# The logits of the second routing: x tiles kept in free places of the weight buffer, one group of twelve tiles, sums written instead of added

## Chip, core and metric

The kernel runs on one core of one Trainium2 chip (trn2). The metric is the device time of one execution in microseconds (us), lower is better. The engines are TensorE (PE, with its weight loads as PEld), VectorE (DVE), ScalarE (ACT), GpSimd (POOL) and SyncE (SP); SP issues most DMAs, POOL all indirect ones.

## What is computed

Attention, then two mixtures of experts, on N = 1536 tokens of D = 512 values, E = 8 experts, FF = 1024 hidden units, all in float32. Only the passage between the two mixtures matters here:

```
x1 = first mixture (each token goes to its two best experts):
     x1[n] = sum over its two experts e of gate[n, e] * (relu(x[n] @ w1[e]) @ w2[e])
second mixture, on x1:
     compute = x1 @ w_skip > 0
     logits  = x1 @ w_gate            (8 per token; with the skip score 9)
     e       = argmax(logits);  gate = softmax(logits)[e]
     out     = x1 + gate * (relu(x1 @ w1'[e]) @ w2'[e])   where compute, else x1
```

So the second routing needs nine numbers of every token of the finished x1, and the second mixture can't gather its first tokens before the lists of that routing are made.

## The kernel before

**Tiling.** P = 128 partitions, NT = 12 tiles of 128 tokens. In the second routing tile t holds the tokens 12p + t (partition p), so a tile is a strided read of x1. Weights of one expert are 16 chunks of 128 x 512 values (WC = 16), cut in PIECES = 8 pieces of 512 KB. SP loads a piece into its place in the buffer `stage` (L571, `load_piece`, at most AIR = 4 in flight), ACT rounds it into `w_hi` (L1097) and DVE subtracts to get `w_lo` (L1615, which counts `s_lo`); only then may that place of `stage` be loaded again. Two sets `w_hi`/`w_lo` alternate. Sets 0 to 7 belong to the first mixture, set 8 is the first of the second mixture and set 9 its second. When the first mixture ends, set 8 is rounded and split, and set 9 lies unrounded in `stage`; it is rounded during the first slots of the second mixture (L1097, L1615 there).

**First mixture.** Experts in order, in rounds of up to W = 416 tokens (parts of 128, 128, 128 and 32); here every expert has one round. A round computes the hidden units (L850), then the output transposed, 128 columns at a time (L856). Each of these four chunks is copied by ACT into `out_t` (L1221), turned back by PE (`turn_y`, L839) and scaled by DVE into `rows_out` (L1855, L1861). In the last expert's rounds `turn_y` also multiplies `out_t` by the second router's weights (L831), which gives the part of the second logits that this last expert adds; DVE scales it into `more_out` (L1844). POOL's `put` sends per round, first, four indirect DMAs of 36-byte rows from `more_out` to the DRAM array `x_more` (L1429, with add), then four of full rows from `rows_out` to `x1_dram` (L1441, with add), and waits for all to land. In rounds of other experts `more_out` is zero.

**The x tiles of the second routing.** Once all experts but the last are put into x1 (wait on `yfree`), SP copies x1 in DRAM to `x_part` (L616, 4 DMAs), lets the last expert's rows be added to `x1_dram` (`s_may_put`), and loads the tiles one by one from `x_part` into `rows_in` (L635), the gather buffer of the first mixture, four places round. That can only start when the last round's gathers are used up, and from tile 4 on each load waits until PE has turned the tile that was there. Before the load of tile 11, SP waits for the sums in `x_more` and loads them as `more_logit` (L631). The last half (4 pieces) of set 9 is loaded after the copy to `x_part`.

**Logits.** For each tile PE turns 128 x 512 values (L1059, 4 transposes into a bank), ACT copies them to `xt_b` (L1174), PE multiplies with the nine router columns as the stationary operand and 128 tokens as the moving one (L768), which gives 9 x 128, ACT copies that to `gt_sb` (L1182) and PE turns it to 128 x 9 (L775). DVE adds `more_logit` (L1683) and runs some 21 small operations (`route`, L1683 to L1766, and `totals`, L1643 to L1653). The order is: PE `ranks` (L786, L791) once `mask_b` (L1723) is there, DVE ranks to lanes and columns, then per tile a lane mask `lane_hot` (DVE L1776, or ACT L1163 and L1156 for the tiles in `by_act`) and `col_val` (DVE L1778), and PE `lists` (L804) sums their product over the tiles. This is done in two groups of six tiles: the first group's DVE work lies beside the logits of the second. ACT stores the gates of each group into x1_dram (L1143), after `s_m1done`, which POOL gives when the first mixture's last rows have landed.

**Start of the second mixture.** DVE casts the lists (L1785), POOL gathers the first slot's rows (L1537, into `xg`), while PE runs ten warm-up matmuls (`keep_warm`, L693); then PE turns the slot (L936), and the matmuls of the slot follow (L964). SP issues four copies of x1 to the output (L642), and POOL the gather of the second slot (L1508). `keep_busy(n, ...)` (L687) is n transposes with no use but to keep PE active.

## Time and profile before

| | us |
|---|---|
| median of 3 runs | 666.77 (666.35 to 667.37) |
| the profiled execution, its own time | 665.87 |
| its span | 663.4 |
| PE busy | 620.8 (94% of the span) |
| DVE busy | 367.9 (55%) |
| ACT busy | 293.9 (44%) |
| POOL busy | 237.9 (36%) |

The span is what the trace covers; the rest of 665.87 lies around it. "Busy" of PE counts matmuls that overlap. In the rows below a time is in us from the start of the span, a mean or a minimum of one instruction in ns. "x4" is a number of instructions, "<-" names who ended an idle time before an instruction.

### The profile page before, as it was taken

To read this page: it belongs to the slowest core of one execution; us is meant where nothing else is said; L and a number is where in the kernel's file an instruction comes from. 1 tells how busy PE (TensorE), PEld (TensorE's weight loads), DVE (VectorE), ACT (ScalarE), POOL (GpSimd) and SP (SyncE) were. 2 spreads that over 40 slices of the span, in tenths; PEclk is the share of its full clock that TensorE was granted. 3 is DMA by queue.
4 is the path that set the end of the run, shared out by engine and by line. 5 is a ranking of instruction groups with operands and counts; after the bars stand their busy time and mean duration, and the time that the engine had idled before them with its cause. 6 is when DMAs were issued, how large, how long until landed. Compare 5 with 4: busy or idle time off the path is not lost.

```text
span 663.4 us, 13555 instructions
## 1 busy us (share of the span) xinstructions
PE 620.8 (94%) x4054; PEld 551.5 (83%) x4054; DVE 367.9 (55%) x714; ACT 293.9 (44%) x536; POOL 237.9 (36%) x223
## 2 busy tenths in 40 slices
PE   6888848999999999999999999998699999999994
PEld 6567735999999999999999999985478888888883
DVE  5759985644535554364644536423564687656641
ACT  2657732433424443253433434433255475646621
POOL 2558303105527063370725527033112223231230
PEclk9999967999999999999999999998699999999998
DMA  9999881442926448283672926885296679568220
GB/s 305 326 285 305 301 295 53 155 152 55 269 66 180 140 93 264 54 213 94 150 207 54 273 65 157 236 251 113 72 330 208 208 220 357 160 187 266 40 50 13
DMA packets 57633, 119.79 MB, mean 181 GB/s; under 512 B 13588, under 2 KB 13972, under 8 KB 57568
## 3 DMA queue, kind: packets, MB, share of 16 engines
q1 hardware_dynamic: 39424, 94.59, 43.4%
q0 software_dynamic: 14304, 23.93, 17.2%
q10 hardware_dynamic: 3840, 0.49, 0.5%
q8 instruction: 30, 0.49, 0.3%
q14 instruction: 35, 0.29, 0.1%
HBM read 103.51 MB, written 23.50 MB: 191 GB/s over the span
## 4 chain that ended last, share of the span: by engine, by line
PE 84%; DMA 5%; DVE 4%; issue 2%; SPq 2%; POOLq 0%; ACT 0%; POOL 0%; DVEq 0%; ACTq 0%
PE bank L964 22%; PE bank L856 22%; PE bank L850 22%; PE bank L839 2%; DMA q_ring<-in_q 2%; PE bank L819 2%; PE bank L745 2%; PE bank L980 2%; PE bank L724 1%; DMA xg<-x_moe,ix_take 1%; PE bank L768 1%; PE bank L758 1%; PE bank L713 1%; PE bank L936 1%; DVE col_val L1778 1%
## 5 line engine op out<-in xcount | busy, mean ns | idle before, releaser
L1615 DVE TENSOR_TENSOR w_lo<-stage,w_hi x120 | 141.7, 1222 | 22.9 <-ACT w_hi L1097 22.1
L1097 ACT CAST w_hi<-stage x120 | 119.7, 1050 | 9.0 <-PE bank L964 8.9
L856 PE MATMUL bank<-unit_hi,w_hi 128*128 128x416 f32 x256 | 92.6, 362 | 0.0
L1873 DVE SCALAR_TENSOR_TENSOR unit_lo<-bank,unit_hi 128x416 fp32r<-128x416 f32 x64 | 37.9, 592 | 96.8 <-ACT unit_hi L1211 96.8
L850 PE MATMUL bank<-tok_hi,w_hi 128*128 128x416 f32 x256 | 90.5, 354 | 0.6 <-DVE tok_lo L1825 0.6
L1211 ACT ACTIVATE unit_hi<-bank 128x416 fp32r<-128x416 f32 x64 | 33.2, 519 | 129.9 <-PE bank L850 129.9
L856 PE MATMUL bank<-unit_lo,w_hi 128*128 128x416 f32 x256 | 90.2, 352 | 0.0
L850 PE MATMUL bank<-tok_hi,w_lo 128*128 128x416 f32 x256 | 89.7, 350 | 0.0
L856 PE MATMUL bank<-unit_hi,w_lo 128*128 128x416 f32 x256 | 89.7, 350 | 0.0
L1429 POOL DMA_INDIRECT x_more<-more_out,ix_put x32 | 51.6, 1614 | 42.2 <-DVE more_out L1844 26.3
L1441 POOL DMA_INDIRECT x_moe<-rows_out,ix_put x32 | 55.2, 1726 | 9.8 <-issue 9.8
L850 PE MATMUL bank<-tok_lo,w_hi 128*128 128x416 f32 x256 | 58.5, 350 | 0.0
L1409 POOL COPY ix_take<-take_ix 128x4 int32 (+1 forms) x8 | 1.5, 184 | 135.2 <-PE bank L819 135.2
L850 PEld LDWEIGHTS bank<-tok_hi,w_hi 128*128 128x128 f32 x256 | 48.0, 188 | 1.5 <-issue 1.0
L856 PEld LDWEIGHTS bank<-unit_hi,w_hi 128*128 128x128 f32 x256 | 48.1, 188 | 1.0
L856 PEld LDWEIGHTS bank<-unit_hi,w_lo 128*128 128x128 f32 x256 | 48.3, 189 | 0.5
L850 PEld LDWEIGHTS bank<-tok_hi,w_lo 128*128 128x128 f32 x256 | 48.1, 188 | 0.4
L856 PEld LDWEIGHTS bank<-unit_lo,w_hi 128*128 128x128 f32 x256 | 48.0, 188 | 0.4
L850 PEld LDWEIGHTS bank<-tok_lo,w_hi 128*128 128x128 f32 x256 | 47.9, 187 | 0.5
L964 PE MATMUL bank<-w_hi,ht_hi 128*128 128x512 f32 x112 | 46.7, 417 | 0.0
L964 PE MATMUL bank<-w_hi,xt_hi 128*128 128x512 f32 x112 | 45.6, 407 | 0.5 <-ACT xt_hi L1254 0.5
L964 PE MATMUL bank<-w_lo,ht_hi 128*128 128x512 f32 x112 | 44.3, 395 | 0.0
(162 smaller groups left out, 1072.5 us busy)
## 6 DMA issues: line engine op xcount, KB each, us to landing
stage<-in_moe_w SPq DMA_DIRECT2D x128, 512.0 KB, 5.6
v_win<-in_v SPq DMA_DIRECT2D x24, 198.0 KB, 8.9
v_raw<-in_v SPq DMA_DIRECT2D x6, 528.0 KB, 13.4
x_moe<-rows_out SPq DMA_DIRECT2D x12, 260.0 KB, 3.6
kt<-in_k SPq DMA_DIRECT2D x8, 384.0 KB, 9.0
q_ring<-in_q SPq DMA_DIRECT2D x6, 512.0 KB, 9.6
x_att<-x_sb POOLq DMA_DIRECT2D x12, 256.0 KB, 5.8
x_part<-x_moe SPq DMA_DIRECT2D x4, 768.0 KB, 8.8
```

The lines of the kernel that those rows point to most:

```text
L745: last = eng.matmul(ps_heads[part, h, 0:HD + 1], pt_sb[:, s % 2, i, part], v_win[:, (2 * t + half) % WR, h * VD:(h + 1) * VD], start=True, ...
L819: last = eng.transpose(ps[:, i * rows:(i + 1) * rows], rows_in[0:rows, t, i * P:(i + 1) * P], ident[0:rows, 0:rows])
L839: last = eng.transpose(ps_turn[0:PART[t], t * P:(t + 1) * P], out_t[:, PSTART[t]:PSTART[t] + PART[t]], ident)
L850: last = eng.matmul(ps_unit[f % 2][:, 0:W], w, x, start=(i == 0), stop=(i == len(mine) - 1))
L856: last = eng.matmul(ps_out[chunk][:, 0:W], w[:, WC // 2 + f, chunk * P:(chunk + 1) * P], h[:, f % UNITS, :], start=(f == 0 and i == 0), st ...
L964: last = eng.matmul(ps[:], *every[i], start=(i == 0), stop=(i == len(every) - 1))
L1097: eng.copy(piece(w_hi[n % SETS], j), stage[:, j, :]).then_inc(s_hi, 1)
L1211: eng.activation(unit_hi[:, f % UNITS, :], ps_unit[f % 2][:, 0:W], ACT.Relu)\
L1429: eng.indirect_dma_start(more_dram, bass.IndirectOffsetOnAxis(ap=ix_put[0:rows, t:t + 1], axis=0), more_out[0:rows, t, :], None, bounds_ch ...
L1441: eng.indirect_dma_start(x1_dram, bass.IndirectOffsetOnAxis(ap=ix_put[0:rows, t:t + 1], axis=0), rows_out[0:rows, t, :], None, bounds_chec ...
L1615: eng.tensor_tensor(piece(w_lo[n % SETS], j), stage[:, j, :], piece(w_hi[n % SETS], j).bitcast(F32), ALU.subtract)\
L1873: eng.scalar_tensor_tensor(unit_lo[:, f % UNITS, :], ps_unit[f % 2][:, 0:W], 0.0, unit_hi[:, f % UNITS, :].bitcast(F32), ALU.max, ALU.subt ...
```

## The change

1. `x_part` is gone, with its four copies. `x1_sb` now lies in places 0 to 5 of `stage` (two tiles in each), which are free from the moment when set 8 is split. SP loads the twelve tiles with six DMAs directly from `x1_dram`, while the last expert's round is computed; `s_may_put` is given when they have landed. Then SP waits for the sums and loads `more_logit`. All eight pieces of set 9 are loaded after that, each of the first six when PE has turned the two tiles in its place.
2. PE turns tiles 0 and 1 in the place of the 8 `keep_busy` transposes ahead of the last `turn_y`; the other 8, behind it, are gone.
3. The logits are computed with the 128 tokens as the stationary operand and the nine router columns as the moving one, straight into 128 x 9. The copy to `gt_sb` and the second turn are gone.
4. One group of twelve tiles instead of two of six; ACT makes `lane_hot` for the six odd tiles, DVE for the even ones. 16 `keep_busy` transposes stand between the last logits and `ranks`.
5. The indirect DMAs to `x_more` write plainly, without add.

```diff
-        ps_rank, ps_list, ps_x1 = bank[1], bank[0], (bank[6], bank[0])
+        ps_rank, ps_list, ps_x1 = bank[1], bank[0], bank[0:2]
...
-        x1_sb = rows_in[:, :, 0:D]
+
+        X1_PIECES = NT * D // (PC * D)
+        x1_sb = stage[:, 0:X1_PIECES, :].rearrange("p j (t d) -> p (j t) d", d=D)
...
-        GROUPS = (((0, NT),), ((0, NT // 2), (NT // 2, NT)))
+        GROUPS = (((0, NT),), ((0, NT),))
...
-        by_act = [2 * t + 1 for t in range(NT)] + [2 * NT + t for t in range(GROUPS[1][1][0], NT, 2)]
+        by_act = [2 * t + 1 for t in range(NT)] + [2 * NT + t for t in range(1, NT, 2)]
...
-            for g in range(PIECES, ready):
-                if g == ready - PIECES // 2:
-                    land(0)
-
...
-                    eng.wait_ge(round_sems["yfree"],
-                                eng.snap(total, min_val=0, max_val=E * ROUNDS) + 1)
-                    for rows in base_rows:
-                        eng.dma_start(part_dram[rows, :], x1_dram[rows, 0:D]).then_inc(s_part, 16)
+            last_set = ready - PIECES
+            for g in range(PIECES, last_set):
                 load_piece(g)
                 land(AIR - 1)
-            eng.wait_ge(s_part, 16 * BASES)
+            land(0)
+
+            eng.wait_ge(s_counted, 1)
+            eng.reg_load(counts, todo_i[0:1, 0:E])
+            eng.reg_mov(total, 0)
+            for e in range(E - 1):
+                eng.reg_add(total, total, counts[e])
+
+            eng.wait_ge(round_sems["yfree"], eng.snap(total, min_val=0, max_val=E * ROUNDS) + 1)
+            by_tile = x1_dram.rearrange("(p t) d -> p t d", t=NT)
+            per = NT // X1_PIECES
+            for i in range(X1_PIECES):
+                eng.wait_ge(s_lo, last_set + i - 2 * PIECES + 1)
+                eng.dma_start(x1_sb[:, i * per:(i + 1) * per, :], by_tile[:, i * per:(i + 1) * per, 0:D])\
+                   .then_inc(s_x1[i], 16)
+            for i in range(X1_PIECES):
+                eng.wait_ge(s_x1[i], 16)
             eng.sem_inc(s_may_put, ROUNDS)
             eng.reg_add(total, total, counts[E - 1])
-            eng.wait_ge(round_sems["xtp"],
-                        eng.snap(total, min_val=0, max_val=E * ROUNDS) * PARTS + (PARTS + 1))
-
-            for t in range(NT):
-                if t == NT - 1:
-
-                    all_rounds = eng.snap(total, min_val=1, max_val=E * ROUNDS)
-                    for part in range(PARTS):
-                        eng.wait_ge(s_put_sums[part], all_rounds * 16)
-                    eng.dma_start(more_logit[:], more_dram.rearrange("(p t) e -> p t e", t=NT))\
-                       .then_inc(s_more, 16)
-                if t >= XR:
-                    eng.wait_ge(s_x1t, t - XR + 1)
-                eng.dma_start(x1_sb[:, t % XR, :], part_dram.rearrange("(p t) d -> p t d", t=NT)[:, t, :])\
-                   .then_inc(s_x1[t % XR], 16)
+            all_rounds = eng.snap(total, min_val=1, max_val=E * ROUNDS)
+            for part in range(PARTS):
+                eng.wait_ge(s_put_sums[part], all_rounds * 16)
+            eng.dma_start(more_logit[:], more_dram.rearrange("(p t) e -> p t e", t=NT)).then_inc(s_more, 16)
+            for g in range(last_set, ready):
+                if g - last_set < X1_PIECES:
+                    eng.wait_ge(s_x1t, (g - last_set + 1) * per)
+                load_piece(g)
+                land(AIR - 1)
...
+            def turn_tile(t):
+                if t % per_piece == 0:
+                    eng.wait_ge(s_x1[t // per_piece], 16)
+                if t >= 2:
+                    eng.wait_ge(s_x1te, t - 1)
+                for i in range(DK):
+                    last = eng.transpose(ps_x1[t % 2][:, i * P:(i + 1) * P],
+                                         x1_sb[:, t, i * P:(i + 1) * P], ident)
+                last.then_inc(s_x1t, 1)

...
             def second_logits(t):

-                if t >= 2:
-                    eng.wait_ge(s_gte, t - 1)
                 for i in range(DK):
-                    last = eng.matmul(gt_place(t)[0:E + 1], wgate2[:, i, :], xt_b[t % 2][:, i, :],
-                                      start=(i == 0), stop=(i == DK - 1))
-                last.then_inc(s_gt[1], 1)
-
-            def turn_logits(t):
-
-                eng.wait_ge(s_gte, t + 1)
-                eng.transpose(second_place(t, t + 1), gt_sb[:, t % 2, :],
-                              ident[0:E + 1, 0:E + 1]).then_inc(s_gl, 1)
+                    last = eng.matmul(second_place(t, t + 1), xt_b[t % 2][:, i, :], wgate2[:, i, :],
+                                      start=(i == 0), stop=(i == DK - 1), skip_group_check=True)
+                last.then_inc(s_gl, 1)
...
-                keep_busy(8, ps_unit[0])
+                for t in range(2):
+                    turn_tile(t)
...
-            keep_busy(8, ps_unit[0])
             eng.wait_ge(s_xt_idle, 1)
-            first, second = GROUPS[1]
-            for t in range(NT + 2):
-                if t < NT:
-                    eng.wait_ge(s_x1[t % XR], 16 * (t // XR + 1))
-                    if t == 2:
-                        eng.wait_ge(s_xt_idle, 2)
-                    if t >= 2:
-                        eng.wait_ge(s_x1te, t - 1)
-                    for i in range(DK):
-                        last = eng.transpose(ps_x1[t % 2][:, i * P:(i + 1) * P],
-                                             x1_sb[:, t % XR, i * P:(i + 1) * P],
-                                             ident)
-                    last.then_inc(s_x1t, 1)
-                if t == first[1] + 4:
-                    ranks(1, first)
-                if 1 <= t <= NT:
+            for t in range(NT):
+                if t >= 2:
+                    turn_tile(t)
+                if t:
                     eng.wait_ge(s_x1te, t)
                     second_logits(t - 1)
-                if t >= 2:
-                    turn_logits(t - 2)
-            lists(1, first)
-            ranks(1, second)
-            lists(1, second)
+            eng.wait_ge(s_x1te, NT)
+            second_logits(NT - 1)
+            eng.wait_ge(s_xt_idle, 2)
+            keep_busy(16, ps_turn)
+            for group in GROUPS[1]:
+                ranks(1, group)
+                lists(1, group)
             second_mixture()
...
-            first, second = GROUPS[1]
             weights(0, GROUPS[0][0])
             store_gates(0, GROUPS[0][0])
             lanes(0, GROUPS[0][0])
             first_mixture()
-            for t in range(NT + 1):
-                if t < NT:
-                    empty_x1(t)
-                if t:
-                    empty_gt(t - 1)
-                if t == first[1] + 3:
-                    weights(1, first)
-
+
+            eng.wait_ge(s_xt_idle, 1)
+            for t in range(NT):
+                empty_x1(t)
+            weights(1, GROUPS[1][0])
             eng.wait_ge(s_m1done, 1)
-            store_gates(1, first)
-            weights(1, second)
-            store_gates(1, second)
-            lanes(1, second)
+            store_gates(1, GROUPS[1][0])
+            lanes(1, GROUPS[1][0])
             second_mixture()
...
-                                               oob_is_err=False, compute_op=ALU.add)\
-                           .then_inc(s_put_sums[t], 16)
+                                               oob_is_err=False).then_inc(s_put_sums[t], 16)
```

## Rows read from the trace of the kernel before

**Rows 1.** The chain of waits in order of time: start, length, what
```profile
438.72 0.59 PE bank L839 x4
...
442.33 0.59 PE bank L1059 x4
442.92 0.97 PE bank L768 x8
...
450.39 5.81 DMA more_logit<-x_more
...
472.66 4.55 PE bank L693 x10
...
479.88 9.24 DMA xg<-x_moe,ix_take
```

**Rows 2.** Timeline of DVE: start, length, line, operation [idle before <-releaser]
```profile
456.31 0.21 DVE L1683 TENSOR_TENSOR logit<-bank,more_logit 128x54 f32<-128x54 f32 x1 [16.11 <-DMA more_logit<-x_more]
...
458.15 0.21 DVE L1723 TENSOR_TENSOR mask_b<-hot,chosen 128x48 bf16<-128x48 f32 x1
...
464.66 0.21 DVE L1683 TENSOR_TENSOR logit<-bank,more_logit 128x54 f32<-128x54 f32 x1 [1.69 <-PE bank L775]
...
468.65 0.17 DVE L1764 SCALAR_TENSOR_TENSOR lane_f<-block_f,rank_f 128x6 f32<-128x6 f32 x1
...
469.65 0.32 DVE L1778 TENSOR_SCALAR col_val<-column_h,col_f,c_late 128x128 f16<-128x128 f16 x1
...
471.26 0.31 DVE L1778 TENSOR_SCALAR col_val<-column_h,col_f,c_late 128x128 f16<-128x128 f16 x1
```

**Rows 3.** Windows: length; PE, PEld, DVE, ACT, POOL busy; then PEclk, DMA share, GB/s
```profile
471.90:477.60 5.70, 4.94 (x15) 3.68 (x14) 1.16 (x4) 0.00 (x0) 1.10 (x1) 0.55 0.17 47
```

**Rows 4.** Timeline of SP: the copies to x_part, all four
```profile
419.42 2.66 SPq L616 DMA_DIRECT2D x_part<-x_moe  x4
```

**Rows 5.** The page's DMA issues: KB each, median us from issue to landing
```profile
stage<-in_moe_w SPq DMA_DIRECT2D x128, 512.0 KB, 5.6
```

**Rows 6.** Timeline of PE in the attention: the first router's logits, and what follows
```profile
47.61 0.96 PE L758 MATMUL bank<-wgate,xt_a 128*128 128x16 f32 x8
48.51 0.69 PE L745 MATMUL bank<-v_win,pt_sb 120*64 120x65 f32 x16
```

**Rows 7.** Timeline of POOL between the mixtures
```profile
440.40 1.56 POOL L1429 DMA_INDIRECT x_more<-more_out,ix_put  x1 [24.02 <-DVE more_out L1844]
...
446.00 1.33 POOL L1429 DMA_INDIRECT x_more<-more_out,ix_put  x1 [0.30 <-issue]
...
453.24 1.33 POOL L1441 DMA_INDIRECT x_moe<-rows_out,ix_put  x1 [0.30 <-issue]
473.28 1.10 POOL L1537 DMA_INDIRECT xg<-x_moe,take_ix  x1 [18.71 <-DVEq L1786]
```

**Rows 8.** POOL's gathers of one line: duration ns min/median/max, first and last start
```profile
L1415 POOL DMA_INDIRECT rows_in<-x_att,ix_take x32: 933/1020/1118, 115.1 to 397.6; - x32
```

**Rows 9.** DVE's reduction of one line at two widths, the same columns
```profile
L1734 DVE TENSOR_REDUCE den<-top_e x2: 202/202/202, 458.5 to 466.8; 128x6 f32<-128x48 f32 x2
L1734 DVE TENSOR_REDUCE den<-gates x1: 252/252/252, 91.8 to 91.8; 128x12 f32<-128x96 f32 x1
```

**Rows 10.** Timeline of DVE, first routing: the first and last of twelve such entries
```profile
96.52 0.53 DVE L1778 TENSOR_SCALAR col_val<-column_h,col_f,c_late 128x128 f16<-128x128 f16 x2
...
103.21 0.52 DVE L1778 TENSOR_SCALAR col_val<-column_h,col_f,c_late 128x128 f16<-128x128 f16 x2
```

**Rows 11.** Timeline of ACT, first routing: its first lanes and the fifth relu
```profile
95.29 0.69 ACT L1163 ACTIVATE lane_hot<-lane_h,lane_f 128x128 f16<-128x128 f16 x2 [4.47 <-DVE lane_f L1764]
...
98.34 0.29 ACT L1156 ACTIVATE lane_hot<-lane_hot 128x128 f16<-128x128 f16 x1
```

**Rows 12.** DMA issues from 445 to 490 us, without a size
```profile
x_moe<-rows_out,ix_put POOLq DMA_INDIRECT x4, 6.7
...
xg<-x_moe,take_ix POOLq DMA_INDIRECT x1, 3.5
```

More of the change, by code:

```diff
@@ L306, in build @@
         col_f = sb_in(routing, "col_f", [P, 2, NT])
-        gt_sb = sb_in(routing, "gt_sb", [E + 1, 2, P])
-        XR = PARTS
         second = ExitStack()
@@ L359, in build @@
         s_xst = [sem(f"s_xst{i}") for i in range(2)]
-        s_gt = [sem(f"s_gt{m}") for m in range(2)]
+        s_gt = sem("s_gt")
         s_z = sem("s_z")
@@ L385, in build @@
         s_lo = sem("s_lo")
-        s_x1 = [sem(f"s_x1{i}") for i in range(XR)]
+        s_x1 = [sem(f"s_x1{i}") for i in range(X1_PIECES)]
         BASES = 4
```

27 lines of the change are left out of this document (6 added, 21 removed).

## Prediction, made before the changed kernel was run

> **What bounds the kernel now.** The page has PE busy for 94% of the span, so inside the two mixtures nothing off PE is worth anything. The change touches only the passage between them, and there I read the chain of waits in order of time [rows 1]. The last turn of the first mixture ends at 438.72 + 0.59 = 439.31 us. Then come eight idle transposes, tiles (0.59 to turn one, 0.97 for its logits), the wait for the sums of the last expert (`more_logit`, issued at 450.39, 5.81 on the way), and more tiles. The timeline of DVE gives the joints [rows 2]: the first group starts at 456.31, when `more_logit` has landed, the second at 464.66, behind the last tile; its last `col_val` ends at 471.26 + 0.31 = 471.57. From there to the second mixture runs a fixed tail: ten warm-ups that end at 477.21 [rows 1], beside the first gather. The passage so far takes 471.57 - 439.31 = 32.3 us, and the question is when the last `col_val` ends. In the tail PE is granted 0.55 of full speed, so mostly the lower level, 1.2 GHz [rows 3], after a stretch in which it waited for DVE; it will wait so again, and I leave the tail as it is.
>
> **Loading the tiles.** The copies to `x_part` start at 419.42 [rows 4], as soon as the rows of the round before the last are in x1. The six new loads wait for the same, and for six pieces of set 8 to be split, which the last round does early. They are as large as weight pieces, 512 KB, of which four in flight take 5.6 us each [rows 5]: six need 8.4 us and are down at 428; at twice that at 436.3. PE asks for tile 0 ahead of the last `turn_y`, at 437. I take no wait; the range allows 1 us. The twelve single loads, and SP's waits for PE among them, go. Moved in exchange: all eight pieces of set 9, four of which were loaded long before, are now issued behind `more_logit`, from about 449. By the same row they need 11.2 us and are down at 460; at twice that at 471.5. Set 9 is first needed in the slots, after that; behind the pieces SP only holds the copies to the output, which wait for the first gather anyway. POOL's queue gets nothing new.
>
> **The turns.** Tiles 0 and 1 take the place of the first eight idle transposes, eight for eight: nothing. The second eight go; what they cost lies ahead of the tiles. ACT empties both tiles beside `turn_y`.
>
> **The tiles.** The second turn and its copy go, a turn stays 0.59. The logits now load 128 columns of tokens and move nine. The nearest row is the first router, tokens stationary with 16 moving columns: its eight instructions hold PE from 47.61 to 48.51, 0.90 us [rows 6]. The old form, 0.97, is the upper bound; below I allow 0.25, as if only the moving columns shrank (0.97 x 9/128 = 0.07) and the rest were starts. With 0.90, 12 x 0.90 + 10 x 0.59 = 16.7 us: the last logits end at 439.31 + 16.7 = 456.0 and DVE can start at 456.05. With 0.97 it is 456.9. The Trainium skill ("TensorE: Matmul & The Clock Gate", Back-to-back issue gap) gives matmuls of up to 64 moving columns some 60 cycles; by that alone a tile's eight cost about 0.2 us, an estimate from that page of the Trainium skill, and the tiles would end near 448. The 0.90 of the first router speaks against it.
>
> **The sums.** The first put to `x_more` starts at 440.40, the fourth at 446.00, 1.87 apart [rows 7]. No plain indirect write is in the trace. Above it is bounded by that put with add; below by POOL's gathers, 1.02 us [rows 8], plus the 0.30 between two. I take the gather, which like the new write has no add: the fourth starts at 440.40 + 3 x 1.32 = 444.4. Landing and SP's step took at most 450.39 - 446.00 = 4.4, and `more_logit` 5.8 (it now shares the DMA engines with pieces instead of tiles): the sums are there at 454.6; with the old pitch at 456.2. So this part by itself is worth at most 0.1; what goes is SP's order, which held `more_logit` behind eleven tile loads.
>
> **One group.** DVE starts once, at 456.05, and not at 464.66: 8.6 earlier. But the work that lay beside the tiles is now bare. The second group took 471.57 - 464.66 = 6.91. Twelve tiles widen some 11 operations from 48 to 96 values per partition, 50 ns each by the two widths of one reduction [rows 9], and two from 90 to 180, some 94 each: 0.74 in all. The masks of six tiles took 471.57 - 469.65 = 1.92; twelve go at the pace of the first routing, where two `col_val` and a `lane_hot` take (103.21 - 96.52) / 11 = 0.61 [rows 10], so 6 x 0.61 = 3.66, or 1.74 more. Sum 6.91 + 0.74 + 1.74 = 9.39, and the last `col_val` ends at 465.4. The 16 idle transposes last at most 4 x 0.59 = 2.4 us, to 458.4; `mask_b` came 2.05 after the start of its group (456.31 to 458.36 [rows 2]) and comes with 0.35 of the widening at 458.45: hidden, barely. A faster tile chain doesn't shift that, as both start together.
>
> **ACT's lanes.** ACT waits for `s_m1done` ahead of the gates and, queued behind them, all six lanes, which PE's lists need (three before, when the rows had long landed). `lane_f` is there at 456.05 + (468.82 - 464.66) + 0.74 = 461.0. In the first routing the fifth relu came 3.05 after the first lane [rows 11]; with a sixth it is some 3.6, so ACT is done at 464.6, with 0.8 to spare. `s_m1done` comes with the last row put, issued at 453.24 [rows 7]; such puts take 6.7 [rows 12]. With quicker sum puts it is issued 1.6 earlier, at 451.6, and lands at 458.3: in time, unless pieces slow it by over 2.7 + 0.8.
>
> **The sum.** 471.57 - 465.44 = 6.1 us less, the tail unchanged. Against the profiled execution: 665.87 - 6.1 = 659.8. The median of the runs is 0.9 above that execution, so the forecast is 666.77 - 6.1 = 660.7. With logits at 0.97, or 1 us lost on a tile, it is 661.6 to 661.7, with both 662.6; with the sums deciding at 454.6, 659.3.
>
> **Rivals.**
> *The pieces get in the way, in part.* They fly from 449 on beside the row puts, the store of the gates and perhaps the first gather (new start 473.28 - 6.1 = 467.2 [rows 7]). For it: the second slot's gather, beside the output copies, took 9.24 [rows 1] where the first took 3.5 [rows 12]. The Trainium skill's rule ("DMA: Bandwidth & Descriptors", Queues, rings and completion order), that each DMA engine goes round the queues that have work, speaks against the change here; those two rows agree with it. Price: a put that lands 5.5 us late costs 2; a gather of 5.5 costs 2. So 662.7 to 664.7. Chance 0.16.
> *The moving columns set the pace* (the case of the Trainium skill's rule): a tile costs 0.59 + 0.25, the tiles end at 448.2, and DVE waits for the sums, 454.6. Gain 6.1 + 1.4 = 7.5: 659.3. For it: so few columns; against it: rows 6. Chance 0.06.
> *Slower: the pieces take over the tail.* At twice their time they fly until 471.5. The last put takes twice its 6.7 and lands at 465.0, the six lanes end at 468.6, 3.2 late, and the first gather takes 9.24, 5.7 more. Together 8.9 against 6.1: 669.6. It decides where such delays pass 6.1. Against it: by their usual time the pieces are down at 460. Chance 0.05.
> *No change.* The bare DVE chain is longer than its sum, or the first tile is late, by the whole 6.1, so that the cover given up equals the start won: 666.8. The first routing, with twice the picks, shows nothing of the kind. Chance 0.03.
>
> **How the numbers follow.** The forecast's own case has 0.70, from 659.3 to 662.6. The range takes in the fast rival with 0.5 for its error and most of the first slow one: 658.8 to 664.2, which leaves out the end of that one, no change, the slower case, and a rest of the own case: 0.2. What a measurement of this kernel can tell from no change is about 0.2%, 1.3 us. Faster by more than that: 0.70 + 0.06 + 0.13 = 0.89; within 0.03 + 0.03 = 0.06; slower 0.05.
>
> **What would show it.** Right: logits at 0.90 a tile, PE without idle to 456; `more_logit` landed before that; one L1683 at 456, its idle ended by PE; puts to `x_more` near 1.0 us each; the last `col_val` at 465.4; the first gather at 467, in 3.5 us. Wrong: L1683 released by a DMA, a first lane on ACT after 461.8, PE waiting for ACT in the lists, or a gather above 5 us.

## The result, and the profile after

The changed kernel took 670.34 us in the median of 11 executions (666.92 to 674.64), the kernel before 665.08 beside it (11 executions, 662.16 to 668.41): ratio 1.0075, 95% interval 1.0052 to 1.0097. That is slower by some 5 us where 6.1 faster was forecast, and outside the range. Ratios here leave out executions more than 1.5% above the fastest of their kernel; that is none of these eleven, but one to three executions in each of five kernels below (`add`, `busy1_add`, `busy2_again`, `busy2_end8`, `early_nine2`), while the medians count all. The profiled execution took 666.92 us, the fastest of the eleven; from its page, and below it the same line of the kernel before:

```profile
span 664.8 us, 13461 instructions
...
PEclk9999967999999999999999999995699999999998
```
```profile
PEclk9999967999999999999999999998699999999998
```

A slice is 664.8 / 40 = 16.6 us; the passage between the mixtures lies in slices 27 to 29 (432 to 482). In slices 28 and 29 the granted clock falls to 5 and 6 tenths, where the kernel before has 8 and 6. The changed kernel in stretches (columns: length; PE, PEld, DVE, ACT, POOL busy; PEclk, DMA share, GB/s):

```profile
440.00:446.00 6.00, 5.59 (x53) 5.36 (x51) 0.00 (x0) 2.34 (x4) 4.63 (x5) 1.00 0.02 2
...
448.00:450.00 2.00, 0.54 (x3) 0.54 (x3) 0.00 (x0) 1.07 (x2) 1.70 (x2) 0.67 0.76 197
450.00:456.00 6.00, 6.00 (x31) 6.00 (x31) 0.00 (x0) 1.17 (x2) 1.95 (x2) 0.50 1.07 334
456.00:462.00 6.00, 6.00 (x31) 6.00 (x31) 0.00 (x0) 1.17 (x2) 0.00 (x0) 0.50 0.70 208
462.00:466.00 4.00, 4.00 (x22) 3.99 (x22) 2.76 (x14) 0.28 (x1) 0.00 (x0) 0.53 0.85 326
```

Up to 446 the clock is 1.00, from 450 to 462 exactly 0.50, the lower of its two levels (1.2 GHz), although PE is busy all of 450 to 462. The chain of waits (start, length, what), against [rows 1]:

```profile
439.01 0.80 PE bank L767 x8
439.80 0.49 PE bank L760 x4
...
445.42 0.41 issue
...
446.88 1.92 PE bank L760 x4
448.82 0.59 ACT xt_b L1157
...
452.28 1.51 PE bank L767 x8
453.79 0.94 PE bank L760 x4
...
462.86 3.27 PE bank L677 x16
...
473.75 4.60 PE bank L683 x10
```

A tile cost 0.80 + 0.49 = 1.29 us at first. Then two waits came (445.42 and, inside the 1.92 of 446.88, the one that ACT's copy at 448.82 ends), and from there 1.51 + 0.95 = 2.46 a tile. ACT's timeline shows the waits from the other side, with what ended its idle time in brackets:

```profile
440.33 0.58 ACT L1157 COPY xt_b<-bank 128x512 f32<-128x512 f32 x1 [1.79 <-PE bank L760]
...
442.98 0.58 ACT L1157 COPY xt_b<-bank 128x512 f32<-128x512 f32 x1 [0.79 <-PE bank L760]
445.19 0.58 ACT L1157 COPY xt_b<-bank 128x512 f32<-128x512 f32 x1 [1.62 <-PE bank L760]
448.82 1.07 ACT L1157 COPY xt_b<-bank 128x512 f32<-128x512 f32 x2 [3.05 <-PE bank L760]
```

ACT waited 3.05 us for a turn that PE had begun at 444.79 and that takes 0.6: the completion reached ACT some 3 us late. The copy before it, at 445.19, was already some 1 us late. DVE, SP and POOL, against [rows 2, 4, 7]:

```profile
462.89 0.27 DVE L1652 TENSOR_TENSOR logit<-bank,more_logit 128x108 f32<-128x108 f32 x1 [22.99 <-PE bank L767]
...
465.10 0.26 DVE L1692 TENSOR_TENSOR mask_b<-hot,chosen 128x96 bf16<-128x96 f32 x1
...
467.88 0.17 DVE L1733 SCALAR_TENSOR_TENSOR lane_f<-block_f,rank_f 128x12 f32<-128x12 f32 x1
...
472.09 0.53 DVE L1747 TENSOR_SCALAR col_val<-column_h,col_f,c_late 128x128 f16<-128x128 f16 x2
```
```profile
417.56 3.18 SPq L612 DMA_DIRECT2D stage<-x_moe  x6
446.10 0.33 SPq L621 DMA_DIRECT2D more_logit<-x_more  x1
446.56 14.52 SPq L562 DMA_DIRECT2D stage<-in_moe_w  x8
```
```profile
440.16 1.03 POOL L1399 DMA_INDIRECT x_more<-more_out,ix_put  x1 [25.36 <-DVE more_out L1813]
...
444.10 0.88 POOL L1399 DMA_INDIRECT x_more<-more_out,ix_put  x1 [0.30 <-issue]
445.28 1.59 POOL L1410 DMA_INDIRECT x_moe<-rows_out,ix_put  x1 [0.30 <-issue]
...
474.32 1.09 POOL L1506 DMA_INDIRECT xg<-x_moe,take_ix  x1 [22.07 <-DVEq L1755]
```

The last `col_val` ends at 472.09 + 0.53 = 472.62, where the forecast had 465.4 and the kernel before 471.57.

The fastest execution understates the loss. Each execution lists its mean granted clock: in the changed kernel's eleven it runs from 0.961 (666.92 us) down to 0.947 (672.11 us) and 0.948 (674.64 us), median 0.951; the kernel before had medians of 0.970 to 0.972 in the later comparisons (21 to 35 executions each). So, on the whole, the executions that lost more time are those that lost more clock.

### The profile page after: what moved, and what is told of

It is laid out like the page before. It is cut to its first block, busy times and chain, and to the rows that moved or that the text cites. A ratio compares the mean times of both kernels' runs of the same rounds, so it can differ in the third digit from the quotient of the medians.

```text
span 664.8 us, 13461 instructions
## 1 busy us (share of the span) xinstructions
PE 622.7 (94%) x4036; PEld 559.4 (84%) x4036; DVE 366.4 (55%) x690; ACT 291.9 (44%) x529; POOL 220.2 (33%) x223
## 4 chain that ended last, share of the span: by engine, by line
PE 87%; DVE 4%; DMA 4%; issue 2%; SPq 1%; ACT 0%; POOLq 0%; POOL 0%; DVEq 0%; ACTq 0%
PE bank L958 22%; PE bank L849 22%; PE bank L843 22%; PE bank L832 2%; PE bank L767 2%; PE bank L812 2%; PE bank L736 2%; PE bank L974 2%; PE bank L715 2%; DMA v_raw<-in_v 2%; PE bank L704 2%; DMA xg<-x_moe,ix_take 1%; PE bank L760 1%; PE bank L749 1%; DVE col_val L1747 1%
## 5 line engine op out<-in xcount | busy, mean ns | idle before, releaser
L1410 POOL DMA_INDIRECT x_moe<-rows_out,ix_put x32 | 59.3, 1852 | 9.8 <-issue 9.8
L1399 POOL DMA_INDIRECT x_more<-more_out,ix_put x32 | 33.3, 1042 | 43.8 <-DVE more_out L1813 27.8
```

The lines of the kernel that those rows point to most:

```text
L1399: eng.indirect_dma_start(more_dram, bass.IndirectOffsetOnAxis(ap=ix_put[0:rows, t:t + 1], axis=0), more_out[0:rows, t, :], None, bounds_ch ...
L1410: eng.indirect_dma_start(x1_dram, bass.IndirectOffsetOnAxis(ap=ix_put[0:rows, t:t + 1], axis=0), rows_out[0:rows, t, :], None, bounds_chec ...
```

## The experiments

The kernels came in five sets, each on one chip beside the kernel before, so ratios can be compared between sets better than medians. None but `plain_pad` is 2% off the kernel before; the differences below are small ones. "Way" is, within the profiled execution, the time from the start of the last expert's logits to the turn of the first slot's rows; it leaves out what the rest of the program does (before: 437.76 to 477.05, with the clock at 0.5 in 460.0 to 463.4, so rather a long one of its kind). "Clock falls" is its first fall behind 430 us. Clock is the median over all executions of their means.

```
kernel        logits  idle  sums   tile us      late   clock  clock  way    median  ratio, 95% interval
              move    /tile        full (half)  comp.  falls  mean   us     us
before        128     0     add    1.71         no     460.0  0.971  39.29  -       1
changed       9       0     plain  1.29 (2.46)  yes    448.7  0.951  40.72  670.34  1.0075 (1.0052-1.0097)
again         9       0     plain  1.28 (2.45)  yes    446.3  0.956  41.06  668.80  1.0054 (1.0031-1.0076)
late          9       0     plain  1.28 (2.45)  yes    447.3  0.957  40.43  668.41  1.0035 (1.0013-1.0057)
moving128     128     0     plain  1.71         yes    468.5  0.972  37.68  665.51  0.9997 (0.9976-1.0018)
busy4         9       4     plain  1.72 (3.31)  yes    453.8  0.953  48.12  675.91  1.0143 (1.0110-1.0177)
nine_only     9       0     add    1.28 (2.45)  no     455.0  0.957  36.65  666.37  1.0009 (0.9983-1.0035)
add           9       0     add    1.28 (2.45)  no     445.7  0.956  38.07  668.63  1.0015 (0.9982-1.0047)
plain_only    128     0     plain  1.71         yes    468.8  0.970  39.09  667.94  1.0027 (1.0000-1.0054)
stage_only    128     0     add    1.71         no     466.0  0.970  35.91  664.23  0.9988 (0.9961-1.0015)
mov_add       128     0     add    1.71         no     471.0  0.971  36.27  664.76  0.9979 (0.9951-1.0007)
stage_early   128     0     add    1.71         no     461.7  0.970  35.89  664.35  0.9993 (0.9957-1.0029)
busy4_add     9       4     add    1.72         no     464.6  0.970  35.98  664.51  0.9983 (0.9955-1.0012)
busy2_add     9       2     add    1.50         no     459.4  0.972  35.06  661.05  0.9931 (0.9904-0.9959)
busy2_again   9       2     add    1.50         no     465.4  0.969  34.76  663.73  0.9946 (0.9913-0.9979)
busy2_end8    9       2     add    1.50         no     460.6  0.968  34.62  663.75  0.9975 (0.9945-1.0005)
busy1_add     9       1     add    1.39         no     465.1  0.956  34.62  669.50  1.0030 (0.9989-1.0070)
early_nine2   9       2     add    1.50         no     460.9  0.961  35.62  665.89  0.9994 (0.9965-1.0023)
plain_pace    128     0     plain  1.71         no     461.9  0.972  40.39  666.93  1.0013 (0.9985-1.0041)
```

(One more, plain_pad, is told below.) `nine_only`, `plain_only` and the two `plain_pa..` are the kernel before with that part alone; `stage_only`, `stage_early` and `early_nine2` keep its two groups.

**First set.** `again` is the changed kernel once more: 

> The changed kernel once more, for a second profile beside its twins of this call. Theory A (the clock): logits with only nine moving columns load PE so lightly that after its first pause the granted clock falls to 1.2 GHz and doesn't come back in the tiles: a tile costs 2.45 us there, 1.29 at 2.4 GHz. It expects the fall again, at about the same place or earlier, and about 670 us, 5 over the kernel before. Theory B (traffic): PE's pause at 447 to 449 us comes from the weight pieces or the plain puts; it expects a pause at the same distance behind the issue of the pieces. Theory C (one group): the bare DVE chain of 9.6 us is the loss, with the clock only a part of it.

`moving128` puts the old logits back:

```diff
-                    last = eng.matmul(second_place(t, t + 1), xt_b[t % 2][:, i, :], wgate2[:, i, :],
+                    last = eng.matmul(gt_place(t)[0:E + 1], wgate2[:, i, :], xt_b[t % 2][:, i, :],
...
+                eng.transpose(second_place(t, t + 1), gt_sb[:, t % 2, :],
```


> The changed kernel with the logits in the old form (nine columns stationary, 128 tokens moving, copy to gt_sb, second turn); tile loads, one group and plain sums stay. Theory A: the clock stays at 2.4 GHz through the tiles, each costs about 1.6 us, the last logits are ready at 439 + 12 x 1.12 + 10 x 0.5 = 457.5 instead of 462.9, and the kernel is 4 to 6 us faster than the changed one, near the kernel before. Theory B: the pause comes all the same and the time stays near 670. Theory C: the same as the changed kernel.

`busy4` adds idle transposes to the changed kernel's tiles:

```diff
                     second_logits(t - 1)
+                    keep_busy(4, bank[3])
```


> The changed kernel with four idle transposes (128 moving columns each, 0.45 us) behind the logits of each of the tiles 0 to 10. Theory A: the clock holds, a tile costs 1.29 + 0.45 = 1.74, the last logits come at 439 + 17.9 + 0.5 = 459 to 460 instead of 462.9, so 3 us or more faster than the changed kernel though PE does more. Theory B and C: the added work of 5 us comes on top, slower than the changed kernel by 3 to 5 us.

`late` holds the pieces of set 9 back until all rows are in x1:

```diff
+            eng.wait_ge(s_m1done, 1)
             for g in range(last_set, ready):
```


> The changed kernel with the eight pieces of set 9 issued only when the first mixture's last rows are in x1 (about 459 us), so none flies beside the tiles before. Theory B: no pause at 447, the clock holds, DVE starts at 456: 6 us faster. Theory A: the same time as the changed kernel within 1 us, with the same fall of the clock.

`late` kept the late completions and the fall of the clock, so the pieces cause neither; what is left to them is at most the step from 1.0054 to 1.0035, within the intervals. They do stretch the last round's row puts: from issue to landing (median of four) 9.4 us in `again` and 5.1 in `late`, against 6.7 before. That held up nothing here, but it comes back in the fourth set. `moving128` kept the clock at 1.00 through all tiles and gave back the whole loss: from 1.0054 to 0.9997, and 3.3 us of the median where 4 to 6 were expected. Yet `busy4`, which has as much for PE to do, was the slowest of all. Its timeline of PE (start, length, line, operation, idle before):

```profile
451.65 0.60 PE L760 MATMUL bank<-c_late,stage 128*128 128x128 f32 x4
453.93 1.88 PE L767 MATMUL bank<-wgate,xt_b 128*128 128x9 f32 x8 [1.68 <-ACT xt_b L1158]
455.65 1.09 PE L677 MATMUL bank<-c_late 128*128 128x128 f32 x4
```

A late completion held PE for 1.68 us there, and the clock fell at the end of that hold, to 0.5 from 453.8 to 477.7, after which the added work cost double. So it could not tell whether work holds the clock; the late completions had to be taken away first.

**Second set, one part at a time.** `nine_only` is the kernel before with the new form of the logits alone (item 3 of the change), `plain_only` with the plain writes alone:

```diff
-                                               oob_is_err=False, compute_op=ALU.add)\
-                           .then_inc(s_put_sums[t], 16)
+                                               oob_is_err=False).then_inc(s_put_sums[t], 16)
```


> The kernel before with one part of the change alone: the logits with tokens stationary and nine columns moving; the copy to gt_sb and the second turn go; two groups, tile loads from x_part, sums with add stay. Theory A (the light logits lose the clock): the granted clock falls in the tile loop here too, a tile costs 2.45 us after it, and the kernel is 2 to 6 us slower than the one before. Theory D (the late completions of PE, seen in all four kernels with tiles in stage and plain sums, lose the clock): without them the clock holds, a tile costs 1.3 to 1.4 us, PE waits for the sums, and the kernel is 0 to 3 us faster than before.

> The kernel before with plain sums alone. POOL's four puts take 1.0 us each in place of 1.56, but more_logit stays behind the tile loads on SP. Theories A and C: no change of the time (within 0.2%). Theory D with the plain writes as cause: PE's completions come up to 3 us late some 8 us after POOL's first put, a tile is held, and the kernel is 1 to 3 us slower than before.

`add` is the changed kernel with that line the other way round, `stage_only` the kernel before with the tiles in the places of weight pieces:

> The changed kernel with the sums added, as before, in place of plain writes. Theory A: the clock falls at 446 to 449 us all the same, time as the changed kernel within 1.5 us. Theory D with the plain writes as its cause: no late completion (ACT's copies of x_b follow PE's turns by less than 1 us), the clock holds, and the kernel is 5 us or more faster than the changed one.

> The kernel before with the tile loads of the change alone (tiles in stage straight from x1, set 9 behind them, more_logit as soon as the sums are there); old logits, two groups, sums with add. more_logit should be there 2 to 4 us earlier than in the kernel before, so the first group's DVE work lies beside the tiles and no tile waits; the clock holds. Theory A: 2 to 4 us faster than before. Theory D with the tiles in stage as the cause of late completions: a hold of 1 to 3 us at tile 5 or 6, and no gain.

Two causes came apart here. In `add` no completion is late and PE has no pause, and the clock falls all the same (windows as above):

```profile
440.00:446.00 6.00, 6.00 (x56) 6.00 (x56) 0.00 (x0) 2.59 (x5) 5.08 (x4) 0.98 0.20 2
446.00:452.00 6.00, 6.00 (x32) 6.00 (x30) 0.00 (x0) 1.76 (x3) 5.06 (x4) 0.50 0.60 114
452.00:459.00 7.00, 7.00 (x36) 7.00 (x36) 0.00 (x0) 1.17 (x2) 1.33 (x1) 0.50 1.06 327
```

PE is busy 100% at 0.50. The Trainium skill ("TensorE: Matmul & The Clock Gate", HAM oscillation) names gaps in which PE idles as what costs the clock; here the trace shows it lost without a gap, with tiles of nine moving columns. Three of `add`'s twelve executions, 671.9 to 674.2 us, are not in its ratio of 1.0015; the mean of all twelve is 668.18 us, beside 665.97 of the kernel before.

And `plain_only`, with the old logits, has the clock but the late completions. DVE's first logits come 19.85 us behind the start of the last expert's logits instead of 18.55 (458.83 - 438.98, 456.31 - 437.76), the second group's no later than before, and the way is no longer. Its ratio of 1.0027 has an interval that reaches 1.0000, so a cost of the plain writes alone is likely, not shown. An estimate: the profile before spent 1.5 us more on three pieces of its last tiles at half clock (1.81 + 0.92 + 1.29 in its chain, against 0.97 + 0.59 + 0.97 at full), which this one did not, so the late completions may have cost about that; in the one-group kernels with the old logits the way is 37.68 with plain and 36.27 with added sums (`moving128`, `mov_add`).

`nine_only` kept full clock from its first logits (442.49) through nine tiles' logits; it fell at 455.0, in a wait of 2.66 us for the ranks, and the last three logits ran at half. `add` lost it 7.5 us behind its first (438.18 to 445.7). So nine columns without filler do not lose the clock at a fixed point. `nine_only` has all sixteen idle transposes ahead of its tiles, two groups and the old loads; which of these held the clock longer was not tested. Over all its executions the mean clock is 0.957, no better than `add`'s 0.956. `stage_only` was expected 2 to 4 us faster: its way is 3.4 shorter, its median 1.3 lower, and its interval holds 1.

**Third set, both undone, or the clock held by work.** `mov_add` is `moving128` with added sums, `busy4_add` is `busy4` with added sums, and `stage_early` is `stage_only` with tiles 0 and 1 turned ahead of `turn_y`:

```diff
-                keep_busy(8, ps_unit[0])
+                for t in range(2):
+                    turn_tile(t)
```


> The changed kernel with the two suspects undone together: logits again with nine stationary and 128 moving columns and a second turn, and the sums again added instead of written; the tile loads from stage, the early turns of tiles 0 and 1 and the one group stay. Theory A (nine moving columns lose the granted clock) and theory D (the plain writes make TensorE's completions late, about 2 us) together: granted clock 1.00 through all tiles, a tile every 1.7 us without a hold, last turn of logits near 460 in a profile of 666, and the median 0.3 to 0.6% below the kernel before, about 662.5. If a pause at tiles 5 and 6 comes in spite of the added sums, D is wrong, and the time is that of the run with the old logits alone, ratio 1.000. Theory G (the one group is the loss, its chain of 9.4 us on VectorE being bare): the clock as above, but a ratio of 1.000 or more, and a kernel with two groups and the same loads is faster by 1 us or more.

> The kernel before with its tiles loaded from stage and, in addition, tiles 0 and 1 turned ahead of the last turn of the expert's result; old logits, two groups, sums added. The run with the loads alone stood at 0.9988. Two tiles of 1.7 us are in work before the loop instead of eight idle transposes: the first group's logits at VectorE about 2 us earlier than in that run where the logits of the expert part are also there (more_logit issued near 450 stays, so the first group's start can't be below 452), the last group's start about 2 to 3 us earlier. Expected ratio 0.994 to 0.998 by theories A and D. Under theory G this one beats the one-group kernel of the same call; under its rival (one group costs nothing, for the first group's ranks and lists lie between the tiles and hold them up) it is the slower of the two or equal.

> The changed kernel with four idle transposes behind the logits of each tile from 0 to 14, as in the earlier run with them, but with the sums added instead of written: the pause at tiles 5 and 6, ahead of which the clock fell in that run, should be gone. If the clock follows how long TensorE works on matrix columns (theory A1), the four transposes of 128 columns take the place of the old logits' 128 moving columns: clock 1.00 through the tiles at about 1.7 us each, last logits near 459, ratio 0.995 to 1.000. If it falls all the same with no pause in the tiles (theory A2: few moving columns behind full weight loads lower it whatever lies between), it stands at 0.5 from about 446 to 454 on, a tile then takes about 3.3 us as in that run, and the ratio is 1.005 to 1.015.

`busy4_add` is the clean form of `busy4`, and the first of the two cases came: clock 1.00 to the last tile.

```profile
446.00:452.00 6.00, 6.00 (x58) 6.00 (x58) 0.00 (x0) 2.04 (x4) 5.08 (x4) 1.00 0.33 29
452.00:459.00 7.00, 7.00 (x68) 7.00 (x66) 0.00 (x0) 2.35 (x4) 3.14 (x3) 1.00 1.03 299
```

All three stand at a way of 35.9 to 36.3 us and 0.998 to 0.999, each with 1 in its interval; `mov_add` and `stage_early` fell short of what was expected of them. Theory G (the one group costs something) seems to get nothing: 35.89 with two groups, 36.27 and 35.98 with one. But these ways can't decide it. ACT and DVE of `stage_early`:

```profile
463.96 0.24 ACT L1141 ACTIVATE top_e<-top_d 128x48 f32<-128x48 f32 x1 [4.15 <-POOLq L1570]
...
464.31 0.20 DVE L1739 TENSOR_REDUCE den<-top_e 128x6 f32<-128x48 f32 x1 [2.05 <-ACT top_e L1141]
```

ACT stores the first group's gates only when the last row put has landed (`s_m1done`, L1570), and `top_e` of the second group stands behind that store. DVE waits 2.05 us for it, and in the kernel before not at all. So the two-group kernel lost 2.0 us there to another wait; without it, an estimate, its way would be some 2 us shorter than that of the one-group kernels. Theory G stays open.

**Fourth and fifth set, less filler, and the late completions.** `busy2_add`, `busy1_add` have two and one transposes in place of four; `busy2_end8` has eight ahead of the ranks instead of sixteen; `busy2_again` repeats `busy2_add`; `early_nine2` puts nine columns and two transposes into `stage_early`.

> As the run before it with four idle transposes behind each tile's logits and added sums (granted clock 1.00 in all tiles, tile 1.72 us, 35.98 us from the last expert's logits to the turn of the first slot's rows), with two transposes instead of four. Theory A1 leaves open how much work holds the clock: with none it fell at 445.7, with four it held. If two hold it, a tile takes about 1.50 us, the last logits end 2.2 us earlier and the stretch is about 33.8 us, ratio 0.993 to 0.997. If two don't, the clock reads 0.5 from somewhere after 446 on, a tile takes 2.9 us from there, and the stretch is 37 to 40 us, ratio 1.000 to 1.006.

> The kernel before with tiles loaded from stage, tiles 0 and 1 turned early, added sums, two groups, nine-moving-column logits and two idle transposes behind the logits of each tile; the first group's ranks stand behind the last turn of a tile. Its sister with the old logits took 35.89 us from the last expert's logits to the turn of the first slot's rows, the one-group form with the same tile pace 35.98. If the clock holds (theory A1, two suffice) a tile takes 1.50 us and the stretch is about 33.5 us, ratio 0.992 to 0.996, provided that the first group's logits at VectorE (not before 451.5, when the sums' logits are read) leave its lists done before the second group's. If the clock falls it is 37 us or more and the ratio 1.000 or above. Theory G (one group costs something of its own) says that it is faster than busy2_add by over 0.5 us in that stretch; its rival says the two agree within 0.5.

> The one-group kernel with nine-column logits, added sums and one idle transpose a tile; with two it had the clock at 1.00 up to 459.4, a tile in 1.50 us and a stretch of 35.06 us, with none the clock fell at 445.7 (38.07 us). Theory A1 (the clock follows how much TensorE has to do): one lies between. If it holds, a tile takes 1.39 us and the stretch is about 34.0, ratio 0.992; if it falls in the midst of the tiles, 36 to 38 us and a ratio of 0.998 to 1.004.

> The faster version with eight idle transposes ahead of the ranks instead of sixteen. In its profile the sixteen took 3.61 us at the lowered clock and ended at about 462.8, 0.76 us after mask_b (462.03). With eight they end by 461.5, and the ranks follow mask_b at once: stretch 34.3 us instead of 35.06, ratio 0.001 below that of its sister in this call. If instead the clock goes down earlier or stays down longer for the missing work, the slot turn is not earlier, and the ratio is that of the sister or above.

> The one-group kernel with nine-column logits, added sums and two idle transposes a tile once more. Its first runs gave 0.9931 with an interval from 0.9904 to 0.9959, and its profile a stretch 4.2 us shorter than that of the kernel before (35.06 against 39.29), of which the start of the second mixture keeps all: 0.9936. So 0.992 to 0.996 again; a value within 0.2% of 1 would say that the first was luck of the runs.

With two the tile is 1.50 and PE has no wait (timeline of PE in `busy2_add`):

```profile
453.00 0.96 PE L767 MATMUL bank<-wgate,xt_b 128*128 128x9 f32 x8
453.82 0.41 PE L677 MATMUL bank<-c_late 128*128 128x128 f32 x2
454.07 0.60 PE L760 MATMUL bank<-c_late,stage 128*128 128x128 f32 x4
...
458.57 0.96 PE L767 MATMUL bank<-wgate,xt_b 128*128 128x9 f32 x8
459.38 3.61 PE L677 MATMUL bank<-c_late 128*128 128x128 f32 x16
462.79 0.24 PE L779 MATMUL bank<-mask_b,before_b 128*128 128x96 bf16 x1
...
476.14 0.81 PE L930 MATMUL bank<-c_late,xg 128*128 128x128 f32 x4 [0.56 <-DMA xg<-x_moe,take_ix]
```

Both sets of executions put it below both kernels, 0.9931 and 0.9946. But it is not safe: three of the twelve executions of `busy2_again`, which its ratio leaves out, took 675 to 676 us at a mean clock of 0.945 to 0.948. The mean of all twelve is 666.07 us, beside 665.71 of the kernel before, so nothing is gained there; in `busy2_add` no execution is left out, and the means are 661.41 and 665.75. With one transpose the profiled execution kept the clock and had a way of 34.62, yet the median of all was 669.50 at 0.956: most lost it.

The ways fell less than the tiles. In `busy2_add` the last `col_val` ends 5.4 us earlier in the way than before (28.40 against 33.81), but the way is only 4.2 shorter, 35.06 where 33.8 was expected. The chain that ended last there no longer runs over PE and DVE:

```profile
456.60 8.75 DMA x_moe<-rows_out,ix_put
...
465.99 5.62 DMA x_moe<-gates
...
472.62 3.48 DMA xg<-x_moe,take_ix
...
476.14 0.82 PE bank L930 x4
```

The last row put lands, only then ACT stores the gates, and the first gather waits for that store. The puts take 9.4 us beside the pieces of set 9 (median of four), so here the pieces do get in the way. `busy2_again`, `busy2_end8` and `busy1_add` have the same chain. That is why `busy2_end8` gained 0.14 us of way, not 0.76 (in `busy2_again`, besides, the sixteen ran at full clock; with eight PE waited 1.64 for `mask_b`); its ratio, 0.9975, is above its sister's and not below. In `early_nine2`, too, the last row put is on the chain: ACT's gates went out at 466.75, and the second group's `top_e` behind them, where its logits had been on DVE at 464.14; those in turn came 3.2 us behind the last tile's (459.90 + 1.04), with the first group's lists between. It was expected at 0.992 to 0.996 and stood at 0.9994. No run held the pieces back in a kernel that kept its clock.

`plain_pad` and `plain_pace` space the plain writes out, with a fill and a drain, or with four fills:

```diff
+                        for k in range(PARTS):
+                            eng.memset(pad[:, t * PARTS + k:t * PARTS + k + 1], 0.0).then_inc(s_pad, 1)
```


> The kernel before with the sums written plainly, as in the earlier run of that part alone (there TensorE's completions came late about 8 us after the first write and the logits reached VectorE 2.5 us later than before), and behind each write a small fill of a spare tile by GpSimd and a drain, so that the writes, and the row writes behind them, are issued about as far apart as the adding ones (1.87 us against 1.32). Theory D1 (the plain writes as such make the completions late): the holds of TensorE in the tiles stay, ratio 1.002 to 1.005. Theory D2 (it is the pace of GpSimd's issues, or the row writes starting earlier): tiles at an even 1.71 us with no hold, ratio 1.000 within 0.2%.

> The kernel before with the sums written plainly and four small fills of a spare tile (one column each) by GpSimd behind each write, with no drain: the four writes of a round should stand 1.7 to 1.9 us apart, as the adding ones do (1.87), instead of 1.32. Theory D1 (plain writes as such make TensorE's completions late): its tiles show holds as in the run with the plain writes alone, logits of the second group at VectorE after 465, stretch from the last expert's logits to the turn of the first slot's rows about 39. Theory D2 (the pace of issue): tiles at 1.71 us without a hold, and the stretch as in a kernel with added sums and the old tile loads, 37.5 to 39.3 us; ratio within 0.2% of 1.000.

`plain_pad` took 697.59 us, ratio 1.0484 (1.0449 to 1.0518): GpSimd stood idle 3 to 5.4 us between a fill and the next write, as if the drain waited for the write to land, so that the last four stood 4.1 to 6.6 us apart (462.36, 468.96, 473.49, 477.57), and it tells nothing of pace. `plain_pace` did not reach its pace either:

```profile
441.58 1.03 POOL L1431 DMA_INDIRECT x_more<-more_out,ix_put  x1 [24.04 <-DVE more_out L1848]
442.56 0.25 POOL L1437 MEMSET pad<- 128x1 f32 x4
442.97 1.01 POOL L1431 DMA_INDIRECT x_more<-more_out,ix_put  x1 [0.16 <-issue]
...
445.68 0.88 POOL L1431 DMA_INDIRECT x_more<-more_out,ix_put  x1 [0.16 <-issue]
...
447.91 1.60 POOL L1445 DMA_INDIRECT x_moe<-rows_out,ix_put  x1 [1.16 <-issue]
```

The writes are still some 1.37 apart (the fills took the place of the 0.30 between two), but the first row write now stands 6.33 behind the first sum, where it stood 5.12 in `plain_only`; and the tiles run at an even 1.71 without a hold (one copy of ACT, at 447.52, came 0.4 late). Its first tile was also late: PE waited 1.13 us for its load, so the tiles stand later beside the writes than in `plain_only`, and the way, 40.39, is outside the 37.5 to 39.3 expected. In this one profile, then, plain writes alone did not make completions late by more than 0.4. All six profiles with them and the row writes right behind had completions some 2 to 3 us late, the twelve with added sums (the kernel before among them) and `plain_pad` had none. Whether it is the row writes' distance, the shifted tiles, or something else in that sequence stays open.

## Why the prediction was wrong

- **Loading the tiles**: right. The six loads went out at 417.56, landed in 3.9 to 7.6 us, and no tile was late. The pieces, issued from 446.56, stretched the row puts from 6.7 to 9.4 us, which here held up nothing (`late`).
- **The tiles**: here the prediction failed. "With 0.90, 12 x 0.90 + 10 x 0.59 = 16.7 us: the last logits end at 439.31 + 16.7 = 456.0" priced all twelve tiles at full clock, from a row in the attention. The price was even too high, 0.80 + 0.49; but the clock fell at 448.7 and the rest cost 2.46. From the end of the last turn (439.01) to the logits on DVE (462.89) it took 23.9 us, 7.1 more than forecast: some 2.5 in the two waits, the rest the halved clock less the 0.2 a tile won. The step counted what the old logits cost PE and not that their 128 moving columns held its clock (`moving128`: 1.00 through all tiles, and the loss gone). The late completions were not needed for the fall: in `add`, without them, it came at 445.7. Whether the idle transposes dropped ahead of the tiles held it too was not tested by itself. Nothing in the prediction priced a fall of the clock ahead of the tail, though the trace of the kernel before has one: behind a wait of 1.78 us for the ranks its clock is 0.50 from 460.0 to 463.4, and there a tile's logits took 1.81 us instead of 0.97:

```profile
460.70 1.88 PE L768 MATMUL bank<-xt_b,wgate 128*9 128x128 f32 x8
```

  The slower rival was another mechanism, and `late` refuted that one: with the pieces held back most of the loss stayed (1.0035 beside 1.0054). The milder one, that the pieces get in the way in part, did not show in the changed kernel, but did in the four one-group kernels with one or two transposes.
- **The sums**: right in price (1.03 + 0.30 against the 1.32 taken; the fourth began at 444.10), and `more_logit` was issued at 446.10, far ahead. That "this part by itself is worth at most 0.1" left out that it may cost: the completions of PE come late with it, 2.5 us of waits in the changed kernel, and alone it stood at 1.0027, just at the edge of its interval.
- **One group**: right in price. DVE's chain took 472.62 - 462.89 = 9.73, against 9.39. Whether two groups would do better with these tiles is open (`stage_early`). That the idle transposes are "hidden, barely" fell with the clock: sixteen took 3.27 and ended 0.8 behind `mask_b` (462.86 + 3.27 against 465.36).
- **ACT's lanes** and the **tail**: right for this kernel, with luck in it. The row puts took 9.4 instead of 6.7, which is 2.7 of the 2.7 + 0.8 of slack named, and nothing in the prediction priced that the first gather waits for the stored gates (5.6 us to land in `busy2_add`); DVE started 6.8 us later than forecast and hid both. The lanes held up nothing, and from the last `col_val` to the end of the warm-ups it took 5.7 us, before 5.6.
- **The sum.** In the profiled execution the way grew by 40.72 - 39.29 = 1.4 us. The medians differ by 5.3, since there most executions had less clock. Against the mildest remedy, `busy4_add` (same parts, added sums, clock held), the way of the changed kernel is 4.7 us longer and the median 5.8. The gain forecast was there to be had in part: 4.2 and 4.5 us of way in the profiled executions with two transposes, and 0.5 to 0.7% of time as long as the clock held.

## What to carry over

Before a matmul with many moving columns is traded for one with few, or idle transposes are dropped, ask what granted the clock: read the granted clock of the stretch, and price the stretch at half speed as well. Filler between short matmuls can be worth more than it costs, here two transposes of 128 columns a tile, though even these lost the clock in three of 22 executions; with one transpose most lost it. When the chain that decided has become shorter, read the chain anew: here the next one, row put, gates, gather, ran over no matmul at all. Take a plain write for an adding one only after a look at what waits for PE's completions while it flies, and judge a kernel near the edge by all its executions, since the profiled one may be the one that kept its clock.

## What the runs showed of the hardware

- PE lost its clock at 100% busy: 0.98 in 440 to 446 and 0.50 from 446 to 459 in `add`, with eight nine-column matmuls and four transposes a tile; with two more transposes a tile (`busy2_add`) it kept 1.00 up to 459.4, through all tiles.
- Completions of PE reached ACT some 3 us late (ACT waited 3.05 at 448.82) about 8 us after the first of four plain indirect writes with row writes right behind; in the profiles of twelve kernels with adding writes never. The cause is open.
- Adding row writes took 9.4 us from issue to landing with eight 512 KB loads in flight beside them (changed kernel), 5.1 with those loads held back (`late`).
- On GpSimd a plain indirect write of the sums took 1.03 to 0.88 us and an adding one 1.56 to 1.33; with a drain behind it GpSimd stood idle 3.0 to 5.4 us before the next (`plain_pad`).
